# Up projections of a two-stage MLP as seven block products, with the weights streamed per group

## The reference

```
x  = attention(q, k, v)                         # window and block sums, 2 x 8 heads
u  = x + (relu(x^T @ w_tok1) @ w_tok2)^T         # 768 -> 256 -> 768 tokens
x  = u + relu(u @ w_ch1) @ w_ch2                 # stage 1: 512 -> 1536 -> 512
xn = (x - mean) / sqrt(var + 1e-6) * g_ln
y  = x + relu(xn @ w2_ch1) @ w2_ch2              # stage 2: 512 -> 2048 -> 512
```

## Time and profile before

| | us |
|---|---|
| median of three runs | 610.54 |
| the profiled execution | 612.84 |
| its span, first to last instruction | 611.1 |
| TensorE busy in the span | 594.0 (97%) |
| VectorE busy | 219.8 (36%) |
| ScalarE busy | 159.4 (26%) |
| GpSimd busy | 49.6 (8%), none of it after the first 109 us |
| mean granted TensorE clock | 0.994 |

### The profile page before, as it was taken

The page is one execution under the profiler, slowest core; times in us unless marked ns, Lnnn a source line. Parts: engine busy times, 40 slices in busy tenths (PEclk is TensorE's granted clock), DMA queues, the critical chain, the costliest instruction groups (busy, mean ns, idle before and its releaser), DMA issues.

```text
span 611.1 us, 7428 instructions
## 1 busy us (share of the span) xinstructions
PE 594.0 (97%) x2808; PEld 484.1 (79%) x2808; DVE 219.8 (36%) x537; ACT 159.4 (26%) x331; POOL 49.6 (8%) x91
## 2 busy tenths in 40 slices
PE   6899999999999999999999999999999999999997
PEld 2677888878888788878888788888788888788886
DVE  5387666466334311134533632112521113211112
ACT  3376664334323101113332310112111102101110
POOL 5356541000000000000000000000000000000000
PEclk9799999999999999999999999999999999999999
DMA  8877532014333000000223100000100000100001
GB/s 231 226 210 225 168 106 96 17 35 137 104 104 104 1 0 1 0 1 8 96 103 104 34 2 2 0 1 0 70 0 1 0 1 0 70 1 0 1 0 69
DMA packets 21305, 35.58 MB, mean 58 GB/s; under 512 B 7596, under 2 KB 7832, under 8 KB 21272
## 3 DMA queue, kind: packets, MB, share of 16 engines
q1 hardware_dynamic: 20720, 34.69, 18.5%
q10 hardware_dynamic: 552, 0.44, 0.3%
HBM read 31.39 MB, written 3.15 MB: 57 GB/s over the span
## 4 chain that ended last, share of the span: by engine, by line
PE 92%; DVE 3%; issue 2%; DMA 2%; ACT 1%; POOL 0%; SPq 0%; DVEq 0%; ACTq 0%; POOLq 0%
PE bank L367 88%; PE bank L516 1%; DMA k_sb<-k_w 1%; DVE neg_scores L725 1%; DMA v_far<-v_mean 1%; PE bank L400 1%; PE bank L402 1%; PE bank L401 1%; DVE k_sb L713 1%; ACT probs L594 0%; DVE natural L844 0%; POOL v_tree L328 0%; ACT tok_w L610 0%; DVE x_split L707 0%; DVE natural L738 0%
## 5 line engine op out<-in xcount | busy, mean ns | idle before, releaser
L820 DVE SCALAR_TENSOR_TENSOR hidden<-bank,hidden 128x512 fp32r<-128x512 f32 x84 | 58.1, 691 | 309.3 <-ACT hidden L644 309.3
L367 PE MATMUL bank<-slots_late,hidden 128*128 128x512 f32 x648 | 156.4, 391 | 0.0
L644 ACT ACTIVATE hidden<-bank 128x512 fp32r<-128x512 f32 x84 | 50.2, 598 | 353.7 <-PE bank L367 353.7
L367 PEld LDWEIGHTS bank<-slots_late,hidden 128*128 128x128 f32 x648 | 120.9, 188 | 24.7
L367 PE MATMUL bank<-in_t,slots_late 128*128 128x512 f32 x576 | 137.7, 389 | 1.1 <-issue 1.1
L367 PEld LDWEIGHTS bank<-in_t,slots_late 128*128 128x128 f32 x576 | 107.9, 188 | 24.5 <-issue 2.3
L367 PE MATMUL bank<-in_t,slots_early 128*128 128x512 f32 x288 | 69.5, 390 | 0.0
L367 PEld LDWEIGHTS bank<-in_t,slots_early 128*128 128x128 f32 x288 | 54.1, 188 | 11.7
L367 PE MATMUL bank<-slots_early,hidden 128*128 128x512 f32 x216 | 51.9, 389 | 0.0
L367 PEld LDWEIGHTS bank<-slots_early,hidden 128*128 128x128 f32 x216 | 40.5, 188 | 8.4
L367 PE MATMUL bank<-k_sb,q_sb 128*128 128x364 f32 x96 | 39.7, 499 | 4.2 <-DVE neg_max L725 2.5
(11 more groups left out here) (72 smaller groups left out, 430.0 us busy)
## 6 DMA issues: line engine op xcount, KB each, us to landing
stage<-w_ch SPq DMA_DIRECT2D x56, 256.0 KB, 2.7
k_sb<-k_w SPq DMA_DIRECT2D x16, 273.0 KB, 4.2
v_own<-v_w SPq DMA_DIRECT2D x8, 390.0 KB, 3.1
q_sb<-q_t SPq DMA_DIRECT2D x8, 384.0 KB, 4.9
v_turned<-v_t SPq DMA_DIRECT2D x8, 384.0 KB, 3.7
out<-natural SPq DMA_DIRECT2D x12, 256.0 KB, 2.1
tok_stage<-w_tok SPq DMA_DIRECT2D x4, 384.0 KB, 4.0
v_far<-v_edge SPq DMA_DIRECT2D x16, 45.0 KB, 2.9
```

The lines of the kernel that those rows point to most:

```text
L367: return nc.tensor.matmul(dst, lhs, rhs, start=start, stop=stop, skip_group_check=True)
L644: nc.scalar.activation(hidden[:, f % HID_RING, 0, :], ch1_bank[f % 2][:, 0:GN], ACT.Relu).then_inc(hid_high, 1)
L820: nc.vector.scalar_tensor_tensor(out=hidden[:, f % HID_RING, 1, :], in0=ch1_bank[f % 2][:, 0:GN], scalar=0.0, in1=hidden[:, f % HID_RING, ...
```

## The change

**Groups and pairs.** A group is now one whole batch of one stage (768 tokens), so there are four groups instead of six. Hidden chunks go in pairs q = 0 to 27 (6, 6, 8 and 8 in the four groups).

**Seven products.** For a pair, the 512x256 block of up weights is seen as 2x2 blocks A (256x128 each) and the group's inputs as 2x2 blocks B (256 channels by 384 tokens). Instead of eight block products there are seven, of A blocks or their sums S1 to S4 with B blocks or their sums T1 to T4. Each product is 6 matmuls of 384 columns. Products 2, 3 and 6 start on a bank that already holds an earlier product. VectorE joins the rest: `u2`, `u3` and three results `c_raw`.

**Who makes what.** GpSimd makes the sums S1 to S4 of each pair (`sum_weights`, four operations of 256 elements), their low part in one operation of 1024 elements (`low_sums`), and the sums T1 to T4 of each group (`sum_inputs`, four of 768). ScalarE copies product 0 (`p1`), makes the high parts of weights, sums and inputs (`high_up`, `high_sums`, `high_down`, `high_input`) and copies the transposed inputs (`copy_batch`). VectorE makes the other low parts (`low_up`, `low_down`, `low_input`).

**Down products.** Down products of pair q - 1 come in twelve units of three matmuls of 512 columns, put between the up products of pair q: 2, 2, 2, 2, 1, 1 and 2 units after products 0 to 6. Each unit adds to one of six accumulator banks, which leaves two banks for up products and transposes.

**Transposes.** A group's inputs are turned in eight batches of three transposes. For group 0 they lie around the token mix of batch 1, for the others at the ends of the pairs that BATCHES_AT names.

**Weights.** No weights are kept: each pair has two loads of 512 KB (up and down), double buffered, split anew in each group. All loops are unrolled.

The diff, cut to what sets the order (`-` lines are mostly left out):

```diff
...
+HT = 3
+HN = HT * P
+PAIRS_OF = (FC[0] // 2, FC[0] // 2, FC[1] // 2, FC[1] // 2)
+FIRST = (0, 6, 12, 20)
...
+B11, T2_, B21, T3_, T1_, T4_, B22 = range(7)
+PRODUCTS = ((B11, A11), (T2_, 3 + S2), (B21, A12), (T3_, 3 + S3), (T1_, 3 + S1), (T4_, A22), (B22, 3 + S4))
+DOWNS_AFTER = (2, 2, 2, 2, 1, 1, 2)
+UNITS = [(t, f) for t in range(NT) for f in range(2)]
+BATCHES = ((0, 0), (0, 1), (1, 0), (1, 1), (2, 1), (3, 1), (2, 0), (3, 0))
+BATCHES_AT = ((2, 2, 2, 2, 0, 0), (0, 0, 2, 3, 3, 0), (0, 0, 2, 2, 2, 2, 0, 0), (0,) * 8)
+T_AT = (4, 5, 6)
+LATE_IN = 4
...
+                sp.dma_start(raw_up[:, q % 2].rearrange("p a c -> p (a c)"), up_v[g // 2][j]).then_inc(ld_up[q % 2], 16)
...
+                if q >= 2:
+                    sp.wait_ge(down_low, q - 1)
+                else:
+                    sp.wait_ge(tok1_done, 2)
+                sp.dma_start(raw_down[:, q % 2], down_v[g // 2][j]).then_inc(ld_down[q % 2], 16)
...
+                tt(sums_up[:, S1], raw[:, A21], raw[:, A22], ALU.add).then_inc(up_sum, 1)
+                pool.wait_ge(up_sum, 3 * q + 1)
...
+            def low_sums(q):
+                pool.wait_ge(up_high, 2 * q + 2)
+                w = up_w[q % 2]
+                nc.gpsimd.tensor_tensor(w[:, 1, 3:7, :], sums_up[:], w[:, 0, 3:7, :].bitcast(F32),
+                                        ALU.subtract).then_inc(sums_low, 1)
...
+            low_sums(1)
+            sum_inputs(0)
+            for q in range(1, NQ):
+                g, j = group_of(q)
+                if q + 1 < NQ:
+                    sum_weights(q + 1)
+                    low_sums(q + 1)
+                if g + 1 < NGROUP and j == T_AT[g]:
+                    sum_inputs(g + 1)
...
+                if (t, f) == (0, 0):
+                    pe.wait_ge(down_low, q + 1)
+                    pe.wait_ge(hid_low, 4 * q + 3)
...
+            def pair(q):
+                g, j = group_of(q)
+                turned = turned_before(q)
+                before = 0 if q == 0 else turned - turned_before(q - 1) if j else 0
+                units = iter(UNITS)
+                for i in range(7):
+                    if i == 0:
+                        pe.wait_ge(raw_low, q + 1)
+                        if q:
+                            pe.wait_ge(c_made, 3 * q - (before == 0))
+                        if q == 0 or before >= 2:
+                            pe.wait_ge(in_copied, turned - 1)
+                    if i == 1:
+                        pe.wait_ge(sums_low, q + 1)
+                        if q:
+                            pe.wait_ge(c_made, 3 * q)
+                        if q == 0 or before:
+                            pe.wait_ge(in_copied, turned)
+                    if i == 2:
+                        pe.wait_ge(p1_copied, q + 1)
+                    if i == 3:
+                        pe.wait_ge(u_made, 2 * q + 1)
+                    if i == 4:
+                        pe.wait_ge(hid_low, 4 * q + 1)
+                    if i == 5:
+                        pe.wait_ge(u_made, 2 * q + 2)
+                    if i == 6:
+                        pe.wait_ge(c_made, 3 * q + 1)
+                    up(q, i)
+                    if q:
+                        for _ in range(DOWNS_AFTER[i]):
+                            down(q - 1, *next(units))
+                for b in range(BATCHES_AT[g][j]):
+                    if g and turned % 8 == 0 and b == 0:
+                        pe.wait_ge(nat_ready, NT * g)
+                    if b < 2:
+                        pe.wait_ge(c_made, 3 * q + 2 + b)
                     else:
+                        pe.wait_ge(in_copied, turned + b - 1)
+                    turn_batch(turned + b)
+
+            for q in range(NQ):
+                pair(q)
+            for t, f in UNITS:
+                down(NQ - 1, t, f)
...
+            def pair(q):
+                g, j = group_of(q)
+                act.wait_ge(up_done, 7 * q + 1)
+                act.wait_ge(u_made, 2 * q)
+                nc.scalar.copy(p1[:], product_bank(q, 0)[:, 0:HN]).then_inc(p1_copied, 1)
+                if j == 0 and g:
+                    for i in range(LATE_IN, 7):
+                        high_input(g, i)
+                if q and q + 1 < NQ:
+                    high_up(q + 1)
+                act.wait_ge(up_done, 7 * q + 3)
+                if q >= 2:
+                    wait_downs(act, q - 2)
+                high_hidden(q, 0, product_bank(q, 2)[:, 0:HN])
+                if q and q + 1 < NQ:
+                    high_sums(q + 1)
+                if g + 1 < NGROUP and j == PAIRS_OF[g] - 1:
+                    high_input(g + 1, 0)
+                    high_input(g + 1, 1)
+                act.wait_ge(c_made, 3 * q + 1)
+                high_hidden(q, 1, c_raw[:, 0])
+                high_down(q)
+                if g + 1 < NGROUP and j == PAIRS_OF[g] - 1:
+                    high_input(g + 1, 2)
+                    high_input(g + 1, 3)
+                act.wait_ge(c_made, 3 * q + 2)
+                high_hidden(q, 2, c_raw[:, 1])
+                act.wait_ge(c_made, 3 * q + 3)
+                high_hidden(q, 3, c_raw[:, 2])
+                if g in (1, 2) and j == 1:
+                    act.wait_ge(ln_step, LN_STEPS * g)
+                    nc.scalar.activation(dev[:], var[:], ACT.Sqrt).then_inc(dev_done, 1)
+                for b in range(BATCHES_AT[g][j]):
+                    copy_batch(turned_before(q) + b)
...
-            inputs_high(0, 0, (0, 1))
-            for w in range(KEPT, KEPT + 2):
-                split(w)
-            inputs_high(0, 0, (2, 3))
-            for w in range(KEPT + 2, 2 * KEPT):
...
+                copy_batch(2 + m)
+            high_input(0, 0)
+            for k in range(4, 8):
+                copy_batch(k)
+            for i in range(1, 7):
+                high_input(0, i)
+            for q in range(NQ):
...
+            def pair(q):
+                g, j = group_of(q)
+                ending = g + 1 < NGROUP and j == PAIRS_OF[g] - 1
+                opening = g > 0 and j == 0
+                dve.wait_ge(up_done, 7 * q + 2)
+                dve.wait_ge(p1_copied, q + 1)
+                nc.vector.tensor_tensor(u2[:], product_bank(q, 1)[:, 0:HN], p1[:], ALU.add).then_inc(u_made, 1)
+                if opening:
+                    for i in range(LATE_IN, 7):
+                        low_input(g, i)
+                if q and q + 1 < NQ:
+                    low_up(q + 1)
+                low_hidden(q, 0, product_bank(q, 2)[:, 0:HN])
+                if opening:
+                    add_out(g - 1, 0)
+                    add_out(g - 1, 1)
+                dve.wait_ge(up_done, 7 * q + 4)
+                nc.vector.tensor_tensor(u3[:], product_bank(q, 3)[:, 0:HN], p1[:], ALU.add).then_inc(u_made, 1)
+                if ending:
+                    low_input(g + 1, 0)
+                    low_input(g + 1, 1)
+                if opening:
+                    add_out(g - 1, 2)
+                dve.wait_ge(up_done, 7 * q + 5)
+                dve.wait_ge(u_made, 2 * q + 2)
+                nc.vector.tensor_tensor(c_raw[:, 0], product_bank(q, 4)[:, 0:HN], u3[:], ALU.add).then_inc(c_made, 1)
+                low_hidden(q, 1, c_raw[:, 0])
+                low_down(q)
+                if opening:
+                    add_out(g - 1, 3)
+                dve.wait_ge(up_done, 7 * q + 6)
+                nc.vector.tensor_tensor(c_raw[:, 1], product_bank(q, 5)[:, 0:HN], u3[:], ALU.add).then_inc(c_made, 1)
+                if ending:
+                    low_input(g + 1, 2)
+                    low_input(g + 1, 3)
+                low_hidden(q, 2, c_raw[:, 1])
+                if opening:
+                    add_out(g - 1, 4)
+                dve.wait_ge(up_done, 7 * q + 7)
+                nc.vector.tensor_tensor(c_raw[:, 2], product_bank(q, 6)[:, 0:HN], u2[:], ALU.add).then_inc(c_made, 1)
+                low_hidden(q, 3, c_raw[:, 2])
+                if opening:
+                    add_out(g - 1, 5)
+                if g in (1, 2) and j == 1:
+                    norm_before(g - 1)
+                if g in (1, 2) and j == 2:
+                    norm_after(g - 1)
...
```

More of the change, by code:

```diff
@@ L46 @@
 KB = 3
+PAD = 640
 AHEAD = 3
@@ L566, in _, with up @@
-            group(0, 0, first=True, fresh=True)
-            with pe.Fori(1, GROUPS - 1) as g:
-                group(0, g)
-            group(0, GROUPS - 1)
-            group(1, 0, fresh=True)
-            with pe.Fori(1, GROUPS - 1) as g:
-                group(1, g)
-            group(1, GROUPS - 1, final=True)
+                if t < 4:
+                    first_batch(4 + t)
+            def up(q, i):
+                g, j = group_of(q)
+                b, a = PRODUCTS[i]
+                dst = up_bank[use[0] % 2][:, 0:HN]
+                use[0] += 1
+                if j == 0:
+                    pe.wait_ge(in_low, 7 * g + i + 1)
+                for c in range(2):
+                    last = three(dst, lambda s: up_w[q % 2][:, s, a, c * P:(c + 1) * P],
```

(25 more changed lines are left out.)

483 lines of the change are left out of this document (250 added, 233 removed).

## The result

The changed kernel takes 664.48 us (median of four runs, 663.58 to 664.86) beside 610.66 for the kernel before on the same chip: a ratio of 1.086, interval 1.084 to 1.088. It is slower, as forecast, but by 54 us where 28 were forecast, and it lies above the range of 617 to 660. The profiled run took 664.86 us, its span is 663.1 and the mean granted clock 0.964, where it was 0.994.

The account below looks back on a forecast made before the run. TensorE was taken as the bound. Waits and lower clock summed to +55.5 us, less 27.3 saved on TensorE: +28.2, giving 641.0 us profiled and 638.7 for the median; range 617 to 660.

Parts of the forecast that it names:

- The sign: Whole kernel: slower than before by 28.2 us, with chance 0.89 of slower.
- The wait for the norm: Pairs 8 and 14: TensorE waits ahead of the first batch for norm_after and its copy, +6.3 us each.
- `c_raw` 0 at the border: Border of groups 1 and 2: late T2 delays c_raw 0, so product 6 waits 4.0 us.
- D: Rival: queued operations cost their distance, not length, so waits are shorter; 623 us, chance 0.15.
- E: Rival: up matmuls take 160 ns with nothing on top of the columns, so not slower; 607 us, chance 0.10.
- B: Rival: up products take 187.5 ns per matmul, another 16.6 us; 655 us, chance 0.17.
- the collision of low parts and sums: VectorE low parts and GpSimd sums wait out each other's operations; +2.0 us over 14 plain pairs.
- C: Rival: the lock, GpSimd blocking VectorE at two or three links in each pair; +9, 647 us, chance 0.08.
- pairs with batches: Eight pairs: batch 1 and the next pair's product 0 wait, 1.5 us each with the lock's delay, +12 us.
- 0.7 us of slack: End of a plain pair: c_raw 1 is ready at 14.7 us, wanted by the next pair's product 0 at 15.44.
- Clock: Two norm waits each bring a stretch at granted clock 0.50, 2.9 us lost each, +5.8 us.
- Start: Token mix and pair 0: first up product 1.25 us later, then pair 0's bare chain; +9.2 us together.

Follow-up runs that it names:

- 4: Changed kernel with the layer norm's square root moved behind high_sums of pair j = 2 and the norm's batches one pair later: 642.01 us.
- 5: Changed kernel with GpSimd's sum_inputs moved ahead of low_sums, nothing left out: 651.17 us.
- experiment 2: Changed kernel with GpSimd's weight sums (from pair 2) and input sums (from group 1) cut to 8 columns, rest left out: 635.32 us.
- 3: Changed kernel with only GpSimd's weight sums cut to 8 columns from pair 2 on, input sums full: 642.57 us.
- Experiment 6: Changed kernel with high_down and low_down moved from behind hidden 1 to behind hidden 0: 634.16 us.
- 7: Changed kernel with three moves together: square root and norm batches later, input sums ahead of low_sums, down splits behind hidden 0: 612.24 us.
- 8: The kernel with the three moves of 7, plus GpSimd's weight sums cut to 8 columns from pair 2 on: 609.11 us.
- experiment 1: Changed kernel with matmuls of zeros added to an accumulator ahead of TensorE's longest waits: 655.13 us.
- Experiment 9: The kernel of 7 with start reordered: low_sums(1), batch copies, input splits 3 to 6, pair 2's sums and low_down(0) all later: 606.4 us.

## Why the prediction came out as it did

**Right.** The sign, and the reason for it: the seven products save what was forecast (174 ns for 173.4 forecast), and hand-ordered links on VectorE, ScalarE and GpSimd give back more. The formula of the Trainium skill (TensorE: Matmul & The Clock Gate, "Back-to-back issue gap") for the gap of a single matmul would have had 162.5 ns for 384 columns; the trace has 174. Loads and longer code cost nothing that shows, as forecast. A plain pair is 15.65 to 15.70 us (15.59 forecast), which is partly luck: 0.15 of the 15.59 was delay, and the plain pair has no gap; its 36 down matmuls at 232 ns instead of 227 make up for it with 0.2 us. The wait for the norm is 5.6 us twice (6.3), for `p1` up to 2.1 (2.3), for `c_raw` 0 at the border 4.3 (4.0), T2 in front of it. Rivals D and E fell with these rows, and B with the 174 ns. The two edits on these waits (4 and 5) came out as expected.

**The step that failed** is the price of the collision of low parts and sums. The mechanism was named, and even called a rival (C, +9, chance 0.08), but it was charged only where it turned out cheap: "some 0.5 us of delay stays within the slack: 0.15 us for each of 14 plain pairs, +2.0", and 0.3 in each of eight pairs with batches. Pairs 4 and 18 were priced as plain ones, and the start and the pairs with the norm had nothing for it; at the borders its term was the late T2. GpSimd's weight sums cost 22 us and its input sums 7 (experiments 2 and 3), lower clock behind the waits included. By place, against my pairs (15.44, and 17.59 with batches; 15.44 + 0.65 + 2.3 + 6.3 with the norm; six of 15.44 and 8.4 at borders; 15.59 for the rest), in us, with the run of experiment 2 in the last column:

| | forecast | measured | excess | sums left out |
|---|---|---|---|---|
| start of pair 1 | 153.1 | 158.5 | 5.4 | 156.1 |
| eight pairs with batches (1-3, 9, 10, 15-17) | 140.7 | 150.1 | 9.4 | 146.3 |
| the pairs with the norm (8, 14) | 49.4 | 53.9 | 4.5 | 49.9 |
| pairs at borders (5, 6, 11, 12, 19, 20) | 101.0 | 111.3 | 10.3 | 95.5 |
| pairs 4 and 18 | 31.2 | 35.7 | 4.5 | 31.5 |
| the other pairs to 26 (eight) | 124.7 | 125.9 | 1.2 | 125.5 |

Where the forecast had a price for the delay, in the pairs with batches and the plain ones, leaving out the sums gives back 3.8 and 0.4 us, for 2.4 and 1.2 forecast. Elsewhere it gives back 4.0 in the pairs with the norm, 15.8 at the borders, 4.2 in pairs 4 and 18 and 2.4 ahead of pair 1. The 15.8 hold the late T2 as well, for which 4.0 was forecast. Rival C had its 9 us in the same cheap places, so its number would have been wrong for the same reason.

The six excesses add up to 35.3; 5.8 of it stood in the sum as clock, which leaves 29.5, where 664.86 - 641.0 = 23.9 is missing. The other 5.6 lie the other way in terms that I can't separate (the loops' issue pieces, the transposes, the end of the run). Some 3 of them may be the price of 226.7 ns, since 360 matmuls of the kernel before took 82.24 us, 228.4 ns each, and its time already holds that: 2016 times 1.7 ns, an estimate.

Three errors made it. First, I took the one hindered row of the kernel before (1202 ns for 685) as the size of any delay, when the longest operation of GpSimd that those rows show beside it is 1.0 us. The delay is up to the length of the operation that is in the way, and the change brought in operations of 1.8 and 2.4 us: a low part of 0.56 took 2.24 and 2.45. In pair 3, where the 0.74 us sums are in the way, it took 0.90 and `low_down` 1.64, which is why those pairs came out. The Trainium skill (SBUF — State Buffer, "Who interferes with whom") has a lock held for a whole operation; the rows agree with it, and it would have given this size had I put GpSimd's lengths in. Second, I set the input sums at 1.80 each and asked only when T2 comes, not what they meet: pairs 4 and 18 had only the 0.15 of a plain pair. They meet hidden 1 and then `low_down`. Third, I gave 0.7 us of slack to a chain in which an operation of 1.2 us, unneeded by anyone until the next pair, stands between two links. Experiment 6 shows that the loss needs both, the hold-up and this place: with `low_down` out of it, three quarters of the hold-up remain and 30 us are gone. Experiments 7 and 8 agree: in the new order, what was worth 22 us is worth 3. How much of that fall is due to `low_down`'s place and how much to the two other moves was not tested.

**Clock.** +5.8 forecast, all behind the two norm waits; 9.4 measured (experiment 1). Pairs 9 and 15, which follow the norm waits, gave only 2.3 and 1.0 of it. The clock also fell behind waits of 2 to 4 us in pairs 0, 8, 11 and others that were not counted.

**Start.** +9.2 forecast, 14.6 by the same points (143.9 to 158.5). 2.3 of it stands ahead of the first up product, which comes at 139.5 instead of 137.25: the last low part of x lay 2.45 us beside GpSimd's `low_sums(1)`. Experiment 9 took that away with four other moves, and 4 us more in pair 0. The 2.3 and the gain of 2.7 there are rough: in the profiled runs of experiments 1 to 8, whose edits hardly touch what stands ahead of it, the first up product came between 138.7 and 141.6.

**Not settled.** How the 29 us of experiment 2 split between longer chains and lower clock: in experiments 2 and 6 the mean clock also rose to 0.978, some 20 us less at the lower level, which by the rate of experiment 1 (9.4 per 35) would be 5 us, an estimate. The 232 ns of down matmuls in rows of six is not explained either; it costs 0.2 us a pair.

## What to carry to other kernels

Put every operation that nobody waits for soon (here the split of the next weights) where its engine idles anyway, never between two links of the chain that feeds the bottleneck; moving it alone took away 30 us of 54 without one operation removed. When work is given to GpSimd, write down the length of each of its operations, and charge that length to any VectorE low part it can meet, since one such meeting can turn 0.56 us into 2.45. If a change saves work on the bottleneck and loses time, the order on the other engines' queues is the first thing to try: here three moves took 664 us to 612, and moves at the start took it on to 604, under the kernel before.
